# A later slot for the product with values, reciprocals at the end of VectorE's slot, and a new order on GpSimd

## The reference

```python
scores = q @ k.transpose(0, 1, 3, 2) / sqrt(64)          # 4 x 8 heads, 576 x 576, d = 64
kth = 32nd largest score of each row
scores = where(scores >= kth, scores, -1e9)
attn = exp(scores - max); attn = attn / (sum(attn) + 1e-9)
x = (attn @ v) as 2304 tokens x 512
gate = sigmoid(x @ w_gate); val = x @ w_val               # 512 x 1536
y = (gate * val) @ w_out                                  # 1536 x 512
h = relu(y @ w_in)                                        # 512 x 2048
out = (h * h) @ w_out2                                    # 2048 x 512
```

## Time and profile before

| | |
|---|---|
| median of 3 runs | 1378.29 us (1376.64 to 1378.45) |
| profiled execution, own time | 1378.71 us |
| its span in the profile | 1376.9 us |
| PE busy | 1240.5 us, 90% of the span |
| VectorE busy | 846.3 us, 61% |
| ScalarE busy | 811.1 us, 59% |
| GpSimd busy | 732.8 us, 53% |
| granted TensorE clock, mean | 0.958 of full speed |
| DMA queue, share of 16 engines | 54.3% |

### The profile page before, as it was taken

The page is one execution under the profiler, slowest core; times in us unless marked ns, Lnnn a source line. Parts: engine busy times, 40 slices in busy tenths (PEclk is TensorE's granted clock), DMA queues, the critical chain, the costliest instruction groups (busy, mean ns, idle before and its releaser), DMA issues.

```text
span 1376.9 us, 20893 instructions
## 1 busy us (share of the span) xinstructions
PE 1240.5 (90%) x6960; PEld 1103.0 (80%) x6960; DVE 846.3 (61%) x1680; ACT 811.1 (59%) x1712; POOL 732.8 (53%) x785
## 2 busy tenths in 40 slices
PE   4555688888689999999999999999999999999999
PEld 3454588887688888888888888888888887889998
DVE  6667777677776666777656768884665686011130
ACT  5677776667776675778656657765555574321130
POOL 5766577677765665687445526854353454122130
PEclk9767799998999999999999999999999999999999
DMA  4666155554465556455555546656454544566665
GB/s 156 230 217 231 63 176 192 180 194 171 158 223 213 207 193 217 167 190 214 206 172 191 187 163 205 211 173 223 152 189 153 190 139 139 168 201 216 218 219 181
DMA packets 78873, 257.73 MB, mean 187 GB/s; under 512 B 8752, under 2 KB 9776, under 8 KB 78768
## 3 DMA queue, kind: packets, MB, share of 16 engines
q1 hardware_dynamic: 78768, 256.41, 54.3%
HBM read 216.01 MB, written 40.37 MB: 186 GB/s over the span
## 4 chain that ended last, share of the span: by engine, by line
PE 69%; POOL 17%; issue 6%; ACT 6%; DMA 2%; SPq 0%; POOLq 0%; ACTq 0%
PE ps L456 17%; PE ps L458 17%; PE ps L457 17%; PE ps L415 10%; POOL below L704 4%; POOL ring L699 4%; PE ps L402 4%; PE ps L390 4%; POOL klo L686 3%; POOL qkh L691 2%; ACT qkh L491 2%; POOL full_buf L765 1%; DMA raw<-qk_in 1%; PE ps L410 1%; ACT below L508 1%
## 5 line engine op out<-in xcount | busy, mean ns | idle before, releaser
L456 PE MATMUL ps<-xy_hi,ring 128*128 128x512 f32 (+2 forms) x800 | 306.1, 383 | 13.6 <-POOL ring L699 6.5
L625 DVE MAX8 top<-work 128x8 f32<-128x576 f32 x432 | 312.1, 750 | 5.0
L458 PE MATMUL ps<-xy_hi,ring 128*128 128x512 f32 (+2 forms) x800 | 298.1, 373 | 0.0
L457 PE MATMUL ps<-xy_lo,ring 128*128 128x512 f32 (+2 forms) x800 | 298.0, 372 | 0.0
L704 POOL TENSOR_TENSOR below<-scores,below 128x576 f32<-128x576 f32 x144 | 206.9, 1437 | 59.1 <-ACT below L508 51.7
L456 PE MATMUL ps<-g_hi,ring 128*128 128x512 f32 (+2 forms) x560 | 212.2, 379 | 9.2 <-POOL ring L699 8.9
L627 DVE MATCH_REPLACE8 work<-top,work 128x576 f32<-128x576 f32 x288 | 213.8, 742 | 0.0
L458 PE MATMUL ps<-g_hi,ring 128*128 128x512 f32 (+2 forms) x560 | 207.5, 370 | 0.0
L457 PE MATMUL ps<-g_lo,ring 128*128 128x512 f32 (+2 forms) x560 | 207.1, 370 | 0.0
L415 PE MATMUL ps<-pt,vt 128*128 128x128 f32 x1440 | 195.0, 296 | 0.0
L415 PEld LDWEIGHTS ps<-pt,vt 128*128 128x128 f32 x1440 | 189.9, 213 | 4.1
(11 more groups left out here) (54 smaller groups left out, 2053.2 us busy)
## 6 DMA issues: line engine op xcount, KB each, us to landing
ring<-w_split SPq DMA_DIRECT2D x273, 512.0 KB, 3.4
w_split<-ring SPq DMA_DIRECT2D x68, 512.0 KB, 2.9
w_raw<-w_in SPq DMA_DIRECT2D x90, 256.0 KB, 3.4
vt<-v_in SPq DMA_DIRECT2D x32, 576.0 KB, 5.6
raw<-qk_in SPq DMA_DIRECT2D x16, 512.0 KB, 5.1
raw<-qk_in SPq DMA_DIRECT2D x16, 416.0 KB, 4.7
raw<-qk_in SPq DMA_DIRECT2D x8, 576.0 KB, 4.5
raw<-qk_in SPq DMA_DIRECT2D x8, 480.0 KB, 4.8
```

The costliest lines, as they stand in the source:

```text
L456: nc.tensor.matmul(dst, w_hi, hi[:, k, 0:WIDTH[c]], start=(k == 0), stop=False)
L457: nc.tensor.matmul(dst, w_hi, lo[:, k, 0:WIDTH[c]], start=False, stop=False)
L458: mm = nc.tensor.matmul(dst, w_lo, hi[:, k, 0:WIDTH[c]], start=False, stop=(k == parts * KT - 1))
L625: nc.vector.max(out=best, in_=sc if step == 0 else wk).then_inc(sel_step[t % 2], 1)
```

## The change

PE's list now has the product with values one slot later (slot `END[u]` + 4), behind the first list of MLP halves, and ahead of the transposes of the next unit. The transposes also move behind the first list of halves. ACT copies the product out after it has enlarged the mask and evacuated the halves of the slot before. VectorE inverts at the end of its slot. On POOL the spreading of the inverse goes from the last third of the turn slot to the very start of the next slot, the mask goes ahead of the sum, and the previous slot's evacuations (with their weight splits) ahead of the normalisation. In slot 23, the first with MLP halves, all six halves go to the third list, since x of chunk 0 now is complete only behind that slot's product.

```diff
@@ shares()
-            a = (len(todo) + 1) // 3
-            b = (len(todo) + 1) // 3
+            a = b = 0 if s == MLP_AT[0] else (len(todo) + 1) // 3
@@ PE
             for s in range(SLOTS):
-                u = UNIT_AT.get(s - TURN)
-                if u is not None:
-                    turn(u)
                 for c, h in SHARES[s][0]:
                     mlp_half(c, h)
+                if s - NORM in UNIT_AT:
+                    times_v(UNIT_AT[s - NORM])
+                if s - TURN in UNIT_AT:
+                    turn(UNIT_AT[s - TURN])
                 if s + 2 < NT:
                     score(s + 2)
                 for c, h in SHARES[s][1]:
                     mlp_half(c, h)
-                if u is not None:
-                    times_v(u)
                 for c, h in SHARES[s][2]:
                     mlp_half(c, h)
@@ ScalarE
-                if s - NORM in UNIT_AT:
-                    copy_pv(UNIT_AT[s - NORM])
                 if 0 <= s - MASK < NT:
                     enlarge(s - MASK)
                 for c, n in blocks_of(SHARES[s - 1][2]) if s else []:
                     evac(c, n)
+                if s - NORM in UNIT_AT:
+                    copy_pv(UNIT_AT[s - NORM])
                 if s - TURN in UNIT_AT:
                     copy_pt(UNIT_AT[s - TURN])
@@ VectorE
-                if s - TURN in UNIT_AT:
-                    invert(UNIT_AT[s - TURN])
                 select_both(s, [2])
                 for c, n in blocks_of(SHARES[s][0] + SHARES[s][1]):
                     evac(c, n)
                 select_both(s, [3])
+                if s - TURN in UNIT_AT:
+                    invert(UNIT_AT[s - TURN])
@@ GpSimd
             for s in range(SLOTS):
+                if s - NORM in UNIT_AT:
+                    spread_inverse(UNIT_AT[s - NORM])
+                if 0 <= s - MASK < NT:
+                    mask(s - MASK)
                 if s - TURN in UNIT_AT:
                     add_eps(UNIT_AT[s - TURN])
+                for c, n in blocks_of(SHARES[s - 1][2]) if s else []:
+                    evac(c, n)
                 if s - NORM in UNIT_AT:
                     normalise(UNIT_AT[s - NORM])
-                if 0 <= s - MASK < NT:
-                    mask(s - MASK)
                 for c, p in X_AT.get(s, []):
                     split_x(c, p)
-                for c, n in blocks_of(SHARES[s - 1][2]) if s else []:
-                    evac(c, n)
-                if s - TURN in UNIT_AT:
-                    spread_inverse(UNIT_AT[s - TURN])
                 for g, h in HEADS_AT.get(s, []):
                     split_head(g, h)
```

## The result

| | before | after |
|---|---|---|
| median | 1378.37 us (1376.64 to 1379.09, 4 runs) | 1461.37 us (1459.79 to 1462.1, 4 runs) |
| span of the profiled execution | 1376.9 us | 1460.0 us |
| granted clock, mean | 0.958 | 0.947 |

The change makes the kernel slower: the ratio is 1.060 (95% interval 1.058 to 1.062). The forecast was 1417 us with a range of 1383 to 1442 us, so the direction was right and the size was off by a factor of two: +83 us where +39 was forecast, outside the range.

A forecast was written before the change was run, and what follows sets the result against it. No engine bounds the opening; PE does after 413 us. Terms +20 + 8 - 7 + 19 + 0 + 1 = +41, taken as +39, gave 1417 us; 8-in-10 range 1383 to 1442 us.

The forecast's parts named there:

- The chain in slot 12: Opening pair slot: spread, product, copy and transposes follow POOL's last weight split in series before the exponential; +5.3 us.
- The opening: Attention-only slots 0 to 22: four pair slots lose +20 us and seven other norm slots +8 us.
- PE's wait for the copy: Pair slots: PE stands still while the product leaves the shared bank, about 0.65 us each; +8 us in chunks 1 to 3.
- the late spread behind head splits: Beside chunk 0: spread 4.0 us later against 1.84 us of cover, about +2 us for 7 pairs; +13 us.
- the named signs: If right: MLP halves start 20 to 30 us later, ACT awaits the product, L410 waits stay behind head splits.
- I take -2.5 us for each of 8: -20: Beside chunk 0, slot pairs without head splits: MLP halves cover PE's wait and the mask comes earlier; -20 us.
- chunk 1: Eleven slots behind head splits stall PE, 0 to 3 us each, since the spread comes late; +14 us.
- stalls and the low clock: Rival: products behind 20 new stalls after 413 us run at the low clock, +29 us; 1446 us, chance 0.14.
- Its price of nothing: Opening: VectorE's 105.4 us wait before the reciprocal goes away as such but is idle time; taken as 0.
- The waits simply go: Rival: the inverse is spread before PE finishes its first list; 1354 us, or 1368 with half the opening's loss; chance 0.14.
- Only the opening loses: Rival: ACT and POOL run far enough ahead in chunks 1 to 3, so +19 us vanish; 1400 us, chance 0.16.
- No change: Rival: beside the opening the orders only trade waits, and the opening's chain is covered; 1378 us, chance 0.06.

The follow-up runs named there:

- a1: The changed kernel with the spread back in GpSimd's turn slot and the reciprocal back in the middle of VectorE's slot; 1379.2 us, ratio 1.002.
- a8: The changed kernel with the spread made by VectorE, directly behind the reciprocal at the end of its slot; 1379.41 us, ratio 1.001.
- b4: The kernel before with only the spread moved, to the start of GpSimd's next slot; 1598.87 us, ratio 1.160.
- a4: The changed kernel with only the reciprocal back in the middle of VectorE's slot; 1464.98 us, ratio 1.062.
- a10: The changed kernel, reciprocal mid-slot on VectorE, spread back in the turn slot only where that slot has a head split; 1394.24 us, ratio 1.011.

## Why the prediction was right in its direction and wrong in its size

**What held.** PE's wait behind GpSimd's list, which the prediction puts first, is the cause (a1, a8, b4). The chain in slot 12 measured 7.6 us from GpSimd's last split to the exponential, where 7.5 was worked out; some luck is in that, since the product took 4.05 us instead of 3.61 and the copies and handovers were shorter by as much. The opening came to +34.4 us, where +28 was taken. In slot 59, for which the prediction took 8.6 us from the start of the transposes to the product, the timeline of the changed kernel has

```profile
499.68 1.17 PE L401 MATMUL ps<-ident,probs_h 128*128 128x128 f32 x9 [0.56 <-ACT rp L533]
508.32 0.30 PE L409 MATMUL ps<-ident,rinv_q 128*128 128x128 f32 x1 [0.96 <-POOL rinv_q L719]
```

which is 8.64 us. All 16 pair slots show PE's wait for the copy (2.3 + 4.7 + 2.3 us in the opening and chunks 1 and 3), 0.56 us or so each, where 0.65 was taken. Chunk 2 was taken at +5 us and measured +11.2. Beside chunk 0, the late spread behind head splits was taken at +13 us; a4 (+16.2 us in that stage) and a10 (+1.2), which differ in that alone, are 15.0 us apart there. Most of the named signs came: the first MLP block came 34 us later, and in the opening ACT waited 52.9 us for the product ahead of its copy. One came only in part. The wait at the transposed inverse (L409) does not stay behind head splits alone: in the opening four units without one have 24.4 of its 80.3 us, since weight splits stand ahead of the spread there too.

**What failed: "I take -2.5 us for each of 8: -20".** This is the largest error, 20.8 us of the missing 44. The prediction had -7 us beside chunk 0, the run +13.8. The step went wrong twice. First, it took the 2.97 us wait of slot 31 for all eight units without a head split. In that slot the cover did work; before and after, the product there reads

```profile
222.82 3.80 PE L415 MATMUL ps<-pt,vt 128*128 128x128 f32 x18
```

```profile
259.73 0.30 PE L409 MATMUL ps<-ident,rinv_q 128*128 128x128 f32 x1
259.87 2.17 PE L414 MATMUL ps<-pt,vt 128*128 128x128 f32 x18
```

But all eight together had waited only 13.4 us, three of them not at all, and the change took that to 5.6 us. The eight with a head split went from 10.8 to 23.1 us, so the total rose from 24.2 to 28.7.

Second, it booked a shorter wait of PE as a shorter stage. The trace of a10 shows why that fails. PE's wait for the spread beside chunk 0 fell there from 24.2 to 7.6 us, but its waits for split weights and their loads rose from 16.0 to 30.9 us (22.9 + 8.0), and the stage is 1.2 us longer than before. In a1, with the wait for the spread down to 3.3 us, the wait for split weights is 25.0 us against 15.4. A wait removed on PE came back as PE's next waits. The prediction names the wait for split weights, and GpSimd's list as part of the pace there, in its first part, and then did not use it. Why the loads come later too is not shown.

**What was mis-sized: chunk 1.** The forecast came to +14 us there, the eleven head splits and the pair slots less the old wait. Measured were +25.4. PE's idle time grew by 19.5 us: 11.0 for the spread (14.2 against 3.2), 4.7 for the copy, and 3.8 for other things, of which I had counted none, such as split weights that come late (2.7), loads (1.6) and a result bank (0.8 us, against 1.2 before). Another 5.9 us are PE's busy time. One reading was also off: the 276.12 us that the prediction divides by the 32 slots of chunk 2 are of 664 to 942 us, which begins in chunk 1. By the stages above, a slot has 8.5 us of PE's busy time in chunk 1 (270.79 / 32) and 8.0 in chunk 2 (254.92 / 32), so PE's own work covers less of the 8.6 us than was taken.

**The clock.** The forecast had the low clock for the opening alone. From the first mark on, PE's busy time for the same matmuls grew by 12.0 us, which is the sign that the prediction names for the clock (more than 10), and by 13.4 us with the opening: less than half of the 29 us of the rival "stalls and the low clock". It is +4.6, +5.9 and +3.3 us in chunks 0 to 2 and -1.8 us in chunk 3, and no term of the sum holds it. That it is the clock is argued and not tested. The granted clock goes with it (0.92 to 0.90 beside chunk 0, 1.00 to 0.99 in chunk 1), and in b4, with 242.7 us of waits for the spread, both went further; but no run holds the clock fixed.

**VectorE.** Its wait ahead of the reciprocal did not go away, as the prediction had it, but rose from 105.4 to 150.0 us. Its price of nothing was right all the same (a4).

**The range.** It did not follow from its own terms. Their upper bounds (+13 beside chunk 0, +54 in chunks 1 to 3, +21 for the other norm slots of the opening) would have covered 1461 us; the range stopped at 1442.

**The rivals.** "The waits simply go" fell: the wait for the spread rose from 53.7 to 131.1 us. "Only the opening loses" fell: 48.7 of 83.1 us are behind it. "No change" fell.

## What to carry to other kernels

A short instruction that another engine waits for belongs as early in its engine's list as its inputs allow, not at a boundary of a slot: in an in-order list, "first in the next slot" means "behind everything of this one". Here a copy of 0.29 us, moved behind the other work of its engine's slot, cost 6% where its reader moved too and 16% where it did not, and moved ahead of the evacuations it gained 1.3%.

When a moved step has its reader moved as well, the time between the two has to be counted on both lists: the reader won two to four MLP halves of cover beside the MLPs and none in the opening, the writer lost a head split, weight splits and remainders. And in a stage in which no engine is full (beside chunk 0 PE was busy for 83% of the time and GpSimd for 71%), a wait that goes is not yet time won: the next wait of that same engine has to be looked up first.

## What the runs showed of the hardware that was not expected

The product of 18 matmuls takes 2.17 us at one level of the clock and up to 4.05 us (slot 12 of the changed kernel) behind a wait of 10.47 us. In slots 28 and 29, PE's wait grew from 1.41 to 2.81 us, and the product behind it went from 2.17 to 3.40 us. The price of a wait can be more than the wait. The length of the wait alone does not tell it: in slot 33 the product took 4.05 us behind a wait of 1.01 us, which followed another of 2.27 us within 3 us, while in slot 59 it took 2.17 us behind a wait of 2.46 us. In the stage of slot 59 (chunk 1) PE is busy for 92% of the time, and its granted clock is 0.99.
